# A fused attention and two-expert-layer kernel: ranks behind the second product, row numbers last, and attention's small steps at other places

## The chip, the cores and the metric

The program runs on one core of a Trainium2 chip. The metric is device time in microseconds (us) of one execution. Engines: PE is the matrix engine (TensorE), DVE is VectorE, ACT is ScalarE, POOL is GpSimd, SP is SyncE, which here only issues DMAs.

## The reference

Three stages run one after the other on 3072 tokens (4 batches of 768) of width 384 (8 heads of 48).

```
f = sigmoid(f_logit)                                  # gated linear attention, per head
state = f[t,:,None] * state + k[t] (x) v[t];  y[t] = q[t] @ state
x = y as rows of 384                                  # first expert layer
logits = normalised x @ normalised expert_emb.T / tau; e = argmax; gate = softmax(logits)[e]
x = gate * (relu(x @ w1[e]) @ w2[e])                  # 8 experts, w1 384x1024, w2 1024x384
skip rows with x @ w_skip <= 0                        # second expert layer: router w_gate,
out = x + gate * (relu(x @ w1b[e]) @ w2b[e])          # else as the first; skipped rows stay x
```

## The kernel before

**Engines and waits.** Each engine runs its own instruction list, written out by hand; semaphores (wait_ge, then_inc) are the only order between engines. An engine that waits holds up all that stands behind it in its list.

**Attention** works on 16 pairs of heads (g = 4b + hp; b is the batch, hp the pair in it), each in a head part and a tail part. PE transposes k, q and f, makes scores (L732) and sums (L718), and multiplies by state (L745) and scores (L753). DVE does the decays (L1171 to L1173, L1184, L1186), k_up (L1179), q_down (L1189) and the running state (L1211). ACT copies and exponentiates. POOL masks the scores (L557), lays out carry (L564), which the state of the next pair needs, and makes the low parts of weights (L550). Between the pairs lies the routing of the batch before. In the tail of hp = 1 DVE normalises and picks the expert (L1273 to L1278: maximum, shifted, tie, first index, onehot_b), and stands there ahead of q_down. In the head of hp = 2 PE counts the ranks (L797 to L802). Then DVE makes row numbers (slot_idx, L1303), and POOL sends the rows to sorted_rows in HBM, by one indirect DMA for each of six chunks (L571). A safety count (ps_safe, L707 and L1208) tells all engines whether a slower exact path must run; with these data it doesn't.

**Weights.** All products of the expert layers are made from a high part (w_hi, ACT, L969) and a low part (w_lo = raw_w - w_hi, POOL, L550) of both operands. The weights of one expert (3 MB) are eight slices of 128x768. There are two buffers. SP loads expert 0 early in attention. Its eight slices are made there, one a pair, in pairs 2, 3, 4, 5, 8, 9, 12 and 13 (first_slice). SP then loads expert 2 into the same buffer, and expert 1 into the other when attention is done, as that buffer lies on attention's memory.

**An expert layer** (m = 0, then m = 1) goes over the experts and over tiles of 128 sorted rows (27 tiles in the first layer, mostly 3 to an expert). One tile on PE, in its order: transposes of xs (L924), the first half of the second product of the tile before (contract, L871 to L873), its router logits (L895), transposes of its second hidden half (L880), the first half of the first product (expand, L861 to L863), **rank of the tile before** (L797, L802), the second half of its second product (contract), transposes of the first hidden half, two thirds of the second half of expand, transposes of row_out of the tile before (route_t, L889), the rest. On DVE: x_lo (L1474), then old_tile of the tile before, which is route_a (L1427 to L1434, its end is onehot_b), hidden_low (h_lo, L1480), place_a (L1442 to L1455: send_row, out_idx, then slot_idx and next_slot from the ranks), finish_a (L1418, L1419: row_out), and last h_lo of the first half of this tile, which the next tile's contract on PE needs. On POOL: two w_lo slices of the next expert, the sends of the tile before (L602, L605), two more slices, and the confirmation that the sends landed, which frees send_row. Slices 0 to 3 fall in an expert's first tile, 4 to 7 in its second, so that four stand in a row from the one tile to the next.

## Time and profile before

| | |
|---|---|
| runs before, us | 795.44, 790.67, 786.24 (median 790.67) |
| profiled execution | 786.7 us, of which 785.0 us are the span of its instructions |
| PE / DVE / ACT / POOL busy, share of span | 89% / 50% / 45% / 50% |
| mean granted clock of TensorE | 0.936 of full |
| attention | 0 to 206 us |
| last routing, plan, first rows back | 206 to 231 us |
| first expert layer | 231 to 537 us |
| its end, plan, first rows back | 537 to 561 us |
| second expert layer | 561 to 785 us |

The span begins with the program's first instruction, and 1.7 us of the time lie outside of it. Busy PE is not the same as PE at its peak: the same instructions take longer where the granted clock is at 0.50 (1.2 GHz) than at 1.00 (2.4 GHz).

### The profile page before, as it was taken

What the parts mean: (1) busy time and instruction counts of PE and PEld (TensorE: products, weight loads), DVE (VectorE), ACT (ScalarE), POOL (GpSimd) and SP (SyncE); (2) the same over time, 40 slices, a digit from 0 to 9 for tenths busy, and PEclk for the clock granted to TensorE, in tenths of its full rate; (3) what the DMA queues carried; (4) which work ended last, traced back from release to release, by engine and by line L of the source; (5) the groups of instructions that cost most, each with busy time, mean ns of one, the idle gap of its engine ahead of it and who ended that gap; (6) DMA issues with size and microseconds to landing.
All of it is one profiled execution on the core that took longest, in us unless ns stands there. A gap on an engine that the chain in (4) does not pass through costs nothing.

```text
span 785.0 us, 16547 instructions
## 1 busy us (share of the span) xinstructions
PE 698.8 (89%) x4912; PEld 628.4 (80%) x4913; DVE 388.7 (50%) x1001; ACT 355.7 (45%) x611; POOL 388.7 (50%) x309
## 2 busy tenths in 40 slices
PE   5889998998719999999999999998399999999992
PEld 4889897997718888788888888887289899898992
DVE  5858988987223554564455555554222222222220
ACT  3556565573205535353534544532254544545420
POOL 4234473543147456563553746641377556658610
PEclk9999999998559999999999999999599999999997
DMA  8675476556530334261423333510454744744110
GB/s 154 158 200 113 83 171 121 129 116 208 188 107 18 126 111 154 86 201 40 134 89 107 129 128 109 179 52 21 152 180 152 228 140 146 229 151 145 51 41 21
DMA packets 147048, 99.42 MB, mean 127 GB/s; under 512 B 109983, under 2 KB 137930, under 8 KB 147008
## 3 DMA queue, kind: packets, MB, share of 16 engines
q1 hardware_dynamic: 140544, 86.19, 38.8%
q0 software_dynamic: 6464, 12.72, 4.5%
q8 instruction: 22, 0.36, 0.2%
q14 instruction: 18, 0.15, 0.1%
HBM read 83.00 MB, written 23.14 MB: 135 GB/s over the span
## 4 chain that ended last, share of the span: by engine, by line
PE 74%; DVE 9%; issue 8%; DMA 3%; ACT 2%; POOL 1%; SPq 1%; ACTq 0%; POOLq 0%; DVEq 0%
PE banks_y L871 9%; PE banks_y L873 8%; PE bank_a L861 8%; PE banks_y L872 8%; PE bank_a L862 8%; PE bank_a L863 8%; PE bank_b L880 5%; PE banks_y L753 4%; PE banks_s L924 2%; PE banks_s L732 2%; PE banks_y L895 2%; PE banks_y L745 2%; DMA raw_f<-in_f_logit 1%; PE banks_y L682 1%; PE banks_s L654 1%
## 5 line engine op out<-in xcount | busy, mean ns | idle before, releaser
L550 POOL TENSOR_TENSOR w_lo<-raw_w,w_hi 128x768 fp32r<-128x768 f32 x128 | 234.0, 1856 | 75.0 <-ACT w_hi L969 68.0
L871 PE MATMUL banks_y<-w_hi,h_hi 128*128 128x384 f32 x384 | 136.4, 355 | 4.7 <-DVE h_lo L1480 4.7
L873 PE MATMUL banks_y<-w_hi,h_lo 128*128 128x384 f32 x384 | 130.5, 340 | 0.0
L872 PE MATMUL banks_y<-w_lo,h_hi 128*128 128x384 f32 x384 | 130.1, 339 | 0.0
L861 PE MATMUL bank_a<-w_hi,x_hi 128*128 128x512 f32 x288 | 127.2, 442 | 3.0 <-DVE x_lo L1474 3.0
L862 PE MATMUL bank_a<-w_lo,x_hi 128*128 128x512 f32 x288 | 115.9, 402 | 0.0
L863 PE MATMUL bank_a<-w_hi,x_lo 128*128 128x512 f32 x288 | 115.8, 402 | 0.0
L1094 ACT ACTIVATE h_hi<-bank_b 128x512 fp32r<-128x512 f32 x96 | 57.4, 598 | 127.7 <-PE bank_b L880 126.5
L1090 ACT ACTIVATE hid<-bank_a 128x512 f32<-128x512 f32 x96 | 57.5, 599 | 106.0 <-PE bank_a L863 104.7
L969 ACT ACTIVATE w_hi<-raw_w 128x768 fp32r<-128x768 f32 x128 | 101.0, 838 | 3.0 <-DMA raw_w<-in_moe_w 3.0
L1480 DVE TENSOR_TENSOR h_lo<-bank_b,h_hi 128x512 fp32r<-128x512 f32 x96 | 66.2, 689 | 61.2 <-ACT h_hi L1094 60.4
L1474 DVE TENSOR_TENSOR x_lo<-banks_s,x_hi 128x384 fp32r<-128x384 f32 x48 | 26.7, 557 | 124.1 <-ACT x_hi L1127 124.1
L602 POOL DMA_INDIRECT sorted_rows<-send_row,slot_idx x28 | 27.7, 989 | 113.1 <-DVE slot_idx L1454 113.1
L871 PEld LDWEIGHTS banks_y<-w_hi,h_hi 128*128 128x128 f32 x384 | 72.7, 189 | 8.0 <-DVE h_lo L1480 6.3
L872 PEld LDWEIGHTS banks_y<-w_lo,h_hi 128*128 128x128 f32 x384 | 72.9, 190 | 0.7
L873 PEld LDWEIGHTS banks_y<-w_hi,h_lo 128*128 128x128 f32 x384 | 72.7, 189 | 0.0
L557 POOL TENSOR_SCALAR_AFFINE_SELECT scores<-scores 128x768 f32<-128x768 f32 x32 | 33.1, 1035 | 78.0 <-ACT scores L1002 78.0
L863 PEld LDWEIGHTS bank_a<-w_hi,x_lo 128*128 128x128 f32 x288 | 55.4, 192 | 13.7
L861 PEld LDWEIGHTS bank_a<-w_hi,x_hi 128*128 128x128 f32 x288 | 55.9, 194 | 12.3 <-DVE x_lo L1474 4.5
L862 PEld LDWEIGHTS bank_a<-w_lo,x_hi 128*128 128x128 f32 x288 | 56.1, 195 | 7.7
L880 PE MATMUL bank_b<-ident,hid 128*128 128x128 f32 x384 | 59.9, 279 | 1.4 <-ACT hid L1090 1.4
L880 PEld LDWEIGHTS bank_b<-ident,hid 128*128 128x128 f32 x384 | 48.8, 149 | 5.2 <-ACT hid L1090 2.8
(183 smaller groups left out, 1105.7 us busy)
## 6 DMA issues: line engine op xcount, KB each, us to landing
raw_w<-in_moe_w SPq DMA_DIRECT2D x32, 1536.0 KB, 7.0
xs<-sorted_rows SPq DMA_DIRECT2D x48, 194.0 KB, 5.1
raw_f<-in_f_logit SPq DMA_DIRECT2D x32, 144.0 KB, 2.7
raw_k<-in_k SPq DMA_DIRECT2D x32, 144.0 KB, 2.9
raw_q<-in_q SPq DMA_DIRECT2D x32, 144.0 KB, 3.1
raw_v<-in_v SPq DMA_DIRECT2D x32, 144.0 KB, 2.9
kept<-sorted_rows SPq DMA_DIRECT2D x21, 194.0 KB
sorted_rows<-pad_row SPq DMA_DIRECT2D x16, 194.0 KB, 2.4
```

The lines of the kernel that those rows point to most:

```text
L550: pool.tensor_tensor(w_lo[par][:, sl, :], raw_w[par][:, sl, :], w_hi[par][:, sl, :].bitcast(F32), ALU.subtract).then_inc(w_split_lo, 1)
L861: pe.matmul(ps_h[half], x_hi[:, kd, :], hi, start=(kd == 0), stop=False)
L862: pe.matmul(ps_h[half], x_hi[:, kd, :], lo, start=False, stop=False)
L863: ins = pe.matmul(ps_h[half], x_lo[:, kd, :], hi, start=False, stop=(kd == KD - 1))
L871: pe.matmul(ps_out, h_hi[:, kf, :], hi, start=(kf == 0), stop=False)
L872: pe.matmul(ps_out, h_hi[:, kf, :], lo, start=False, stop=False)
L873: ins = pe.matmul(ps_out, h_lo[:, kf, :], hi, start=False, stop=(kf == KF - 1))
L880: ins = pe.transpose(ps_ht[half][:, j * P:(j + 1) * P], hid[:, half * HALF + j * P:half * HALF + (j + 1) * P], ident[:])
L969: act.activation(w_hi[par][:, sl, :], raw_w[par][:, sl, :], ACT.Copy).then_inc(w_split_hi, 1)
L1090: act.activation(hid[:, half * HALF:(half + 1) * HALF], ps_h[half], ACT.Relu).then_inc(s[f"relu{half}"], 1)
L1094: act.activation(h_hi[:, half * (KF // 2):(half + 1) * (KF // 2), :].rearrange("p k x -> p (k x)"), ps_ht[half], ACT.Copy).then_inc(s[f"h_ ...
L1480: dve.tensor_tensor(h_lo[:, hs, :].rearrange("p k x -> p (k x)"), ps_ht[half], h_hi[:, hs, :].bitcast(F32).rearrange("p k x -> p (k x)"), ...
```

## The change

Nothing is added or taken away in what is computed; steps are put at other places.

- **First expert layer.** PE makes the second half of the second product ahead of the ranks, not behind them. On DVE the onehot goes behind h_lo, out of route_a into place_a; the row numbers become a function of their own, place_slot, that stands behind finish_a; next_slot is made ahead of slot_idx. PE's router logits now also wait for place_slot of the tile before, as both use one bank. The semaphore of row numbers starts at one, so POOL waits for u + 2 in place of u + 1 (the same event).
- **Attention.** The high slices go to pairs 3, 4, 7, 8, 11, 12, 14, 15, the low ones to 3, 4, 8, 12, and the last four to the end, ahead of the last batch's sends. SP loads expert 1 ahead of expert 2. The six sends of a batch stand as 2 behind carry (hp = 2), 2 between the masks and 2 behind carry (hp = 3), in place of 3 and 3 ahead of carry. The norm of the expert embedding (ACT and DVE, pair 1) is begun earlier. The safety count moves behind the sums of the last pair and into another bank.

```diff
@@ order in the program, pools and waits @@
-        ps_safe = bank_y[0:1, 448:449]
+        ps_safe = bank_a[0:1, 448:449]
...
-            return g - 2 if b == 0 and hp >= 2 else 2 * b + hp if b > 0 and hp < 2 else None
+        HI_PAIRS = (3, 4, 7, 8, 11, 12, 14, 15)
+        LO_PAIRS = (3, 4, 8, 12)
@@ SP @@
+            sp.wait_ge(y_ready, PAIRS)
+            load_w1(0, 1, 1)
+            load_w2(0, 1, 1)
             wait_split(sp, 0, 2)
             load_w1(0, 2, 0)
             load_w2(0, 2, 0)
-            sp.wait_ge(y_ready, PAIRS)
-            load_w1(0, 1, 1)
-            load_w2(0, 1, 1)
@@ POOL @@
                 mask(g, 0)
+                if b > 0 and hp == 3:
+                    send_chunks(b - 1, (2, 3), (b - 1) % 2)
                 mask(g, 1)
-                if b > 0 and hp >= 2:
-                    send_chunks(b - 1, range((hp - 2) * (C // 2), (hp - 1) * (C // 2)), (b - 1) % 2)
-                if first_slice(g) is not None:
-                    split_lo(0, 0, first_slice(g))
+                if g in LO_PAIRS:
+                    split_lo(0, 0, LO_PAIRS.index(g))
                 if g + 1 < PAIRS:
                     carry_decay(g + 1)
+                if b > 0 and hp >= 2:
+                    send_chunks(b - 1, (0, 1) if hp == 2 else (4, 5), (b - 1) % 2)
+            for sl in range(len(LO_PAIRS), SLICES):
+                split_lo(0, 0, sl)
             send_batch(B - 1, (B - 1) % 2)
@@ PE @@
-                if last:
-                    pe.wait_ge(safe_ready, 1)
-                    pe.matmul(ps_safe, safe_b[:], ones[:, 0:1], start=True, stop=True).then_inc(safe_summed, 1)
...
                 else:
+                    pe.wait_ge(safe_ready, 1)
+                    pe.matmul(ps_safe, safe_b[:], ones[:, 0:1], start=True, stop=True).then_inc(safe_summed, 1)
                     logits(KD * B - 2, ps_logit_end)
...
                     pe.wait_ge(g["xt_copied"], k + 1)
+                    pe.wait_ge(g["slot"], k + 1)
...
+                    pe.wait_ge(s["h_lo1"], u + 1)
+                    contract(par, 1).then_inc(s["y"], 1)
                     if m == 0:
                         rank(g, u + 1, 1, ps_rank_1, ps_count_1)
-                    pe.wait_ge(s["h_lo1"], u + 1)
-                    contract(par, 1).then_inc(s["y"], 1)
@@ ACT: emb_sq in the head of pair 1, its root ahead of the wait for y_ready; split_hi in HI_PAIRS @@
...
@@ DVE @@
             def place_a(ch, k):
+                first_i, valid = cols[:, 1, 0:1], cols[:, 4, 0:1]
                 dve.tensor_scalar(onehot_b[:, 0, :], order[:, 0, :], first_i, valid, ALU.is_equal, ALU.mult).then_inc(g["onehot"], 1)
...
+            def place_slot(ch, k):
+
+                g = gs[1]
                 dve.wait_ge(g["onehot"], k + 1)
                 dve.wait_ge(g["rank"], k + 1)
...
+                ch.link(dve.tensor_tensor(next_slot[:, 0, :], next_slot[:, 0, :], ps_count_1[:, 0, :], ALU.add))
                 dve.tensor_scalar(slot_idx[:, 0:1], cols[:, 3, 0:1], BIG, None, ALU.add).then_inc(g["slot"], 1)
-                ch.link(dve.tensor_tensor(next_slot[:, 0, :], next_slot[:, 0, :], ps_count_1[:, 0, :], ALU.add))
...
                         hidden_low(1, u)
                         place_a(ch, u)
                         finish_a(ch, u)
+                        place_slot(ch, u)
```

How the instructions stand in a row, at the three places that matter. DVE, first expert layer, a tile's work for the tile before, in the kernel before (cols holds the small columns, tie the marks of the best expert):

```order
L1433 TENSOR_REDUCE cols<-tie 128x1
...
L1434 TENSOR_SCALAR onehot_b<-order,cols 128x8
L1480 TENSOR_TENSOR h_lo<-bank_b,h_hi 128x512
L1442 TENSOR_SCALAR cols<-cols 128x1
...
L1446 COPY send_row<-row_out 128x388
...
L1451 TENSOR_TENSOR slot_e<-banks_y,next_slot 128x8
...
L1454 TENSOR_SCALAR slot_idx<-cols 128x1
...
L1419 TENSOR_SCALAR row_out<-banks_y,kept 128x384
```

The same piece of the changed kernel:

```order
L1488 TENSOR_TENSOR h_lo<-bank_b,h_hi 128x512
L1444 TENSOR_SCALAR onehot_b<-order,cols 128x8
L1446 TENSOR_SCALAR cols<-cols 128x1
...
L1450 COPY send_row<-row_out 128x388
...
L1423 TENSOR_SCALAR row_out<-banks_y,kept 128x384
L1459 TENSOR_TENSOR slot_e<-banks_y,next_slot 128x8
...
L1462 TENSOR_TENSOR next_slot<-next_slot,banks_y 128x8
...
L1463 TENSOR_SCALAR slot_idx<-cols 128x1
```

The onehot has moved behind h_lo, and the row number behind row_out. On POOL, the pairs 5, 6 and 7 of attention with carry of the next pair behind each, before:

```order
L557 AFFINE_SELECT scores<-scores 128x768 x2
L550 TENSOR_TENSOR w_lo<-raw_w,w_hi 128x768
L564 COPY carry<-decay 128x48x5
L557 AFFINE_SELECT scores<-scores 128x768 x2
L571 DMA sorted_rows<-rows,slot_idx 25600x388 x3
L564 COPY carry<-decay 128x48x5
L557 AFFINE_SELECT scores<-scores 128x768 x2
L571 DMA sorted_rows<-rows,slot_idx 25600x388 x3
L564 COPY carry<-decay 128x48x5
```

and after:

```order
L555 AFFINE_SELECT scores<-scores 128x768 x2
L562 COPY carry<-decay 128x48x5
L555 AFFINE_SELECT scores<-scores 128x768 x2
L562 COPY carry<-decay 128x48x5
L569 DMA sorted_rows<-rows,slot_idx 25600x388 x2
L555 AFFINE_SELECT scores<-scores 128x768
L569 DMA sorted_rows<-rows,slot_idx 25600x388 x2
L555 AFFINE_SELECT scores<-scores 128x768
L562 COPY carry<-decay 128x48x5
L569 DMA sorted_rows<-rows,slot_idx 25600x388 x2
```

The slice of pair 5 is gone, and carry stands ahead of the sends. On POOL at the end of attention, after (before, nine sends stood there in a row behind the last masks, three of batch 2 and six of batch 3, and no slice):

```order
L569 DMA sorted_rows<-rows,slot_idx 25600x388 x2
L548 TENSOR_TENSOR w_lo<-raw_w,w_hi 128x768 x4
L569 DMA sorted_rows<-rows,slot_idx 25600x388 x6
```

Four slices now stand between the masks of the last pair and the sends of the last batch.

## Rows read from the trace of the kernel before

**Rows 1.** Windows: stretch, length, busy by engine, granted clock, DMA share, GB/s.

```profile
0.00:206.00 206.00, 184.59 (x2030) 173.86 (x2031) 156.69 (x257) 109.92 (x161) 88.99 (x106) 0.93 0.61 141
206.00:231.00 25.00, 5.18 (x33) 4.50 (x33) 7.92 (x41) 2.69 (x6) 5.84 (x6) 0.50 0.54 193
231.00:537.00 306.00, 291.48 (x1683) 256.66 (x1682) 157.67 (x547) 140.62 (x275) 166.18 (x116) 0.98 0.33 108
138.65:142.06 3.41, 3.41 (x19) 3.41 (x19) 3.24 (x7) 0.81 (x1) 1.51 (x3) 0.50 0.05 19
```

**Rows 2.** Waits: who waited for whom, us in total, times, longest.

```profile
PE banks_y L797 <- DVE onehot_b L1434: 10.7, 8, 1.4
PE banks_s L732 <- DVE q_down L1189: 5.9, 4, 1.8
```

**Rows 3.** Windows of single tiles, from one tile's xs transposes to the next's.

```profile
262.71:273.45 10.74, 10.74 (x65) 9.60 (x64) 5.87 (x21) 6.56 (x12) 5.80 (x5) 1.00 0.58 200
273.45:287.78 14.33, 12.60 (x65) 11.15 (x64) 7.65 (x21) 6.44 (x12) 11.12 (x8) 0.88 0.43 141
343.99:356.73 12.74, 11.01 (x66) 9.63 (x65) 7.65 (x21) 6.44 (x12) 9.53 (x7) 1.00 0.48 154
```

**Rows 4.** Timeline of POOL and DVE, tiles that begin at 262.71 and 273.45.

```profile
265.50 3.64 POOL L550 TENSOR_TENSOR w_lo<-raw_w,w_hi 128x768 fp32r<-128x768 f32 x2 [3.71 <-ACT w_hi L969]
266.93 0.43 DVE L1434 TENSOR_SCALAR onehot_b<-order,cols 128x8 bf16<-128x8 f32 x1
268.25 1.11 DVE L1446 COPY send_row<-row_out 128x388 f32<-128x388 f32 x1
273.25 7.21 POOL L550 TENSOR_TENSOR w_lo<-raw_w,w_hi 128x768 fp32r<-128x768 f32 x4
277.54 2.95 DVE L1434 TENSOR_SCALAR onehot_b<-order,cols 128x8 bf16<-128x8 f32 x1
```

**Rows 5.** Timeline, the same tiles: send, row_out, h_lo, PE behind them, h_hi.

```profile
270.97 0.99 POOL L602 DMA_INDIRECT sorted_rows<-send_row,slot_idx  x1 [1.83 <-DVE slot_idx L1454]
271.04 0.62 DVE L1419 TENSOR_SCALAR row_out<-banks_y,kept 128x384 f32<-128x384 f32 x1
271.85 0.69 DVE L1480 TENSOR_TENSOR h_lo<-bank_b,h_hi 128x512 fp32r<-128x512 f32 x1 [0.19 <-issue]
272.43 0.49 PE L889 MATMUL banks_s<-ident,row_out 128*128 128x128 f32 x3
273.70 0.42 PE L871 MATMUL banks_y<-w_hi,h_hi 128*128 128x384 f32 x1
277.12 0.60 ACT L1094 ACTIVATE h_hi<-bank_b 128x512 fp32r<-128x512 f32 x1 [1.03 <-PE bank_b L880]
```

**Rows 6.** Groups of the first layer: instructions, then busy us, mean ns, idle before.

```profile
L1452 DVE TENSOR_TENSOR slot_e<-slot_e,onehot_b 128x8 f32<-128x8 f32 x26 | 4.3, 167 | 0.9
```

**Rows 7.** Timeline of attention: tie beside POOL's slice (pair 5), and tie alone.

```profile
80.92 1.85 POOL L550 TENSOR_TENSOR w_lo<-raw_w,w_hi 128x768 fp32r<-128x768 f32 x1 [0.36 <-ACT w_hi L969]
81.13 1.70 DVE L1276 SCALAR_TENSOR_TENSOR tie<-shifted,order 128x48 f32<-128x48 f32 x1
214.43 0.21 DVE L1276 SCALAR_TENSOR_TENSOR tie<-shifted,order 128x48 f32<-128x48 f32 x1
```

**Rows 8.** Timeline of attention: pair 7's state, the last pair's safety count.

```profile
101.39 0.76 DVE L1211 TENSOR_TENSOR_SCAN state<-banks_y,carry 128x288 f32<-128x288 f32 x1 [1.42 <-POOL carry L564]
190.46 0.17 PE L707 MATMUL banks_y<-ones,safe_b 128*1 128x1 bf16 x1 [0.75 <-DVE safe_b L1336]
```

**Rows 9.** Timeline of pair 2: the embedding's transposes and the next f.

```profile
36.02 0.32 PE L810 MATMUL banks_y<-ident,emb_n 8*128 8x8 f32 x3 [2.18 <-DVE emb_n L1244]
46.56 1.51 PE L654 MATMUL banks_s<-ident,raw_f 128*128 128x128 f32 x6 [2.91 <-DMA raw_f<-in_f_logit]
```

**Rows 10.** Timeline of the first layer's end.

```profile
546.99 0.97 POOL L605 DMA_INDIRECT out<-send_row,out_idx  x1 [0.30 <-issue]
550.82 0.36 DVE L1446 COPY send_row<-row_out 128x388 f32<-128x388 f32 x1
```

More of the change, by code:

```diff
@@ L249, in gla_moe_program @@
         from_one_act = [y_copied, exact_copied]
-        from_one_dve = [exact_done, gs[0]["slot"], gs[0]["onehot"], exact_gs["slot"], exact_gs["onehot"]] + [
+        from_one_dve = [exact_done, gs[0]["slot"], gs[0]["onehot"], exact_gs["slot"], exact_gs["onehot"], gs[1]["slot"]] + [
             f[n] for f in fs for n in ("x_lo", "row")]
@@ L598, in send_routed @@
             def send_routed(u):
-                pool.wait_ge(gs[1]["slot"], u + 1)
+                pool.wait_ge(gs[1]["slot"], u + 2)
                 settle(pool)
@@ L820, in _ @@
             pe.wait_ge(gs[0]["logit_read"], KD * B - 1)
+            pe.wait_ge(safe_known, 1)
             logits(KD * B - 1, ps_logit_end)
@@ L990, in pair_head @@
                     guess_decay(g + 1)
+                if g == 1:
+                    act.wait_ge(small_in, 32 + 32 * KD)
+                    act.activation(emb_sq[:], emb_rows[:], ACT.Square, accum_out=en[:, 0:1]).then_inc(emb_sq_ready, 1)
             def copy_x(r):
@@ L1019, in pair_tail @@
                     square(g - 1)
-                if first_slice(g) is not None:
+                if g in HI_PAIRS:
                     act.wait_ge(w1_in[0], 16)
                     act.wait_ge(w2_in[0], 16)
-                    split_hi(0, 0, first_slice(g))
+                    split_hi(0, 0, HI_PAIRS.index(g))
                 if f_next:
@@ L1027, in pair_tail @@
                     copy_x(x_part(g))
+                if g == 1:
+                    act.wait_ge(emb_norm_ready, 1)
+                    ach.link(act.activation(en[:, 2:3], en[:, 1:2], ACT.Ln))
+                    act.activation(en[:, 3:4], en[:, 2:3], ACT.Exp, scale=0.5).then_inc(emb_sq_ready, 1)
                 act.wait_ge(y_ready, g + 1)
@@ L1033, in pair_tail @@
                                ACT.Copy).then_inc(y_copied, 1)
-                if g == 1:
-                    act.wait_ge(small_in, 32 + 32 * KD)
-                    act.activation(emb_sq[:], emb_rows[:], ACT.Square, accum_out=en[:, 0:1]).then_inc(emb_sq_ready, 1)
-                    act.wait_ge(emb_norm_ready, 1)
-                    ach.link(act.activation(en[:, 2:3], en[:, 1:2], ACT.Ln))
-                    act.activation(en[:, 3:4], en[:, 2:3], ACT.Exp, scale=0.5).then_inc(emb_sq_ready, 1)
             def root(s, b):
@@ L1161, in _ @@
             ROUTE_A = 19
-            TILE_STEPS = (10, 1)
+            TILE_STEPS = (11, 1)
             starts = lambda t: t[:].rearrange("p (c x) -> p c x", c=C)[:, :, 0]
@@ L1205, in pair_head @@
                     place_ranks(ch, gs[0], b - 1)
-                if last:
-                    dve.wait_ge(safe_summed, 1)
-                    dve.tensor_copy(safe_count[:], ps_safe).then_inc(safe_known, 1)
                 dve.wait_ge(u_ready, g + 1)
@@ L1217, in pair_tail @@
                     scale_k(ch, g + 1, 1 - par)
+                if g == 1:
+                    dve.wait_ge(emb_sq_ready, 1)
+                    dve.tensor_scalar(en[:, 1:2], en[:, 0:1], TINY, None, ALU.max).then_inc(emb_norm_ready, 1)
                 if hp == 1 and b > 0:
@@ L1228, in pair_tail @@
                     add_logits(ch, KD * B - 2, ps_logit_end)
+                    dve.wait_ge(safe_summed, 1)
+                    dve.tensor_copy(safe_count[:], ps_safe).then_inc(safe_known, 1)
                 if g == 1:
@@ L1433, in route_a @@
                 ch.link(dve.tensor_reduce(first_i, tie[:, 0, :], AX.X, ALU.min))
-                dve.tensor_scalar(onehot_b[:, 0, :], order[:, 0, :], first_i, valid, ALU.is_equal, ALU.mult).then_inc(g["onehot"], 1)
             def place_a(ch, k):
                 g, total = gs[1], cols[:, 2, 0:1]
-                valid = cols[:, 4, 0:1]
+                first_i, valid = cols[:, 1, 0:1], cols[:, 4, 0:1]
+                dve.tensor_scalar(onehot_b[:, 0, :], order[:, 0, :], first_i, valid, ALU.is_equal, ALU.mult).then_inc(g["onehot"], 1)
                 dve.wait_ge(g["exp"], k + 1)
@@ L1446, in place_a @@
                 dve.tensor_copy(send_row[:], row_out[:])
-                dve.scalar_tensor_tensor(out=out_idx[:], in0=valid, scalar=BIG, in1=row_out[:, TOKEN:TOKEN + 1],
-                                         op0=ALU.mult, op1=ALU.add)
+                ch.link(dve.scalar_tensor_tensor(out=out_idx[:], in0=valid, scalar=BIG, in1=row_out[:, TOKEN:TOKEN + 1],
+                                                 op0=ALU.mult, op1=ALU.add))
+            def place_slot(ch, k):
+                g = gs[1]
                 dve.wait_ge(g["onehot"], k + 1)
@@ L1511, in _ @@
                     place_a(ch, last)
+                    place_slot(ch, last)
                     make_plan(ch, 1)
```

4 lines of the change are left out of this document (removed).

## Prediction

> **What bounds the kernel now.** I read the stages first, then who waits for whom, then single tiles. In attention PE is busy 185 of 206 us, in the first expert layer 291 of 306 us [rows 1], so PE is the bound in both, and what the change can win there is PE's idle time and its time at the low clock. Between the two lie 25 us in which PE does little. In the second expert layer the order is as before, and I count nothing. Two waits carry the rest: PE's ranks for the onehot, 10.7 us in 8 times, and the scores for q_down, 5.9 us in 4 times [rows 2]. A usual tile of the first layer takes 10.74 us, a second tile of an expert 12.74 us, and 14.33 us where the clock falls after the wait [rows 3].
>
> **Why the onehot is late.** It takes 0.43 us in a first tile and 2.95 us in a second [rows 4]; the second case comes seven times. The reader is to see where it ends: at 277.54 + 2.95 = 280.49, while POOL's four w_lo slices run from 273.25 to 280.46. The slices are four of 1.8 us, so it began 0.7 us into the third, was not let in at that one's end (278.66), and was held until the fourth's. In the first tile it began 0.4 us before the first of two slices ended and got in there (267.36); the copy into send_row was then held until the second ended (269.14, and it ended at 269.36). So DVE's onehot and send_row wait for POOL's slices, whereas h_lo doesn't. In the order before, h_lo stands behind the onehot, and PE waits for both.
>
> **Second tiles, seven times.** With the new order h_lo needs only h_hi, which ends at 277.72 [rows 5], so it is done by 278.4, ahead of PE, which comes to the ranks at 279.1 or so. The 2.0 us of wait (12.74 - 10.74) go. What is late next? place_slot is five linked steps of 0.2 us [rows 6], and now stands behind row_out. So the row number comes some 2.3 us later than before, and POOL's sends, which follow it, begin at about 273.5 in place of 270.97 [rows 5] and end at about 275.8. The four slices shift with them, to 275.8 to 283.0, with ends at 277.6, 279.4, 281.2 and 283.0. The onehot begins at 278.4, 0.8 us into the second slice, nearest to the case at 277.54. By that row it is held through the third (281.2). send_row then begins at 281.6 and is held to 283.0, and row_out, which in a usual tile ends 8.95 us after the tile's start (271.66 for 262.71), ends at 284.2, 10.8 us after it. PE wants row_out for route_t 9.7 us after the start (272.43) and waits 1.1 us. Behind row_out come place_slot and h_lo, which PE wants 11.0 us after the start (273.70); that is late by another 0.3 us. The new stall is 1.4 us, the gain 0.6 us a tile, **4.2 us** in seven. The ends of this: 0.1 us a tile if the onehot is held to the last slice's end, 2.0 us if DVE is let in at every end, so 0.7 to 14 us. Two of the seven stalls are followed by a stretch at the low clock, 14.33 - 12.74 = 1.6 us each; I take one of them as gone, **1.6 us** (0 to 3.2).
>
> The Trainium skill (SBUF — State Buffer, "Who interferes with whom") says that VectorE in a 2-port mode and GpSimd lock each other out for the whole instruction, and that the one that issues first has the ports. By that rule the onehot would get in at 278.66. The row of 2.95 us speaks against it, and the row of 0.43 us for it; by the rule alone the gain would be the full 14 us. It is the first rival below.
>
> **Other tiles, 19 of them.** h_lo of the first half begins 0.81 us after row_out began (271.04, 271.85) and is done at 272.54; PE wants it at 273.70. place_slot pushes it by 0.85 us, to 273.4 [rows 5, 6]. That leaves 0.3 us, and costs nothing. If place_slot took more, each tile would pay.
>
> **The layer's end.** place_slot of the last tile but one now comes after row_out, so its two sends go out 2.8 us later than at 546.99 (the first of them starts 1.3 us ahead) [rows 10]. Their landing frees send_row, which DVE writes at 550.82. The send at 546.99 could take until then, 3.8 us, and 2.3 us are near what lies between; with 549.8 + 2.3 the copy starts at 552.1 or later. Plan and first rows follow, and the new order of next_slot adds 0.2: **-1.6 us** (0 to -2.8).
>
> **Attention, pairs 5, 9 and 13.** tie takes 1.70 us beside POOL's slice and 0.21 us alone [rows 7], and stands ahead of q_down, for which PE then waits 1.8 us, three times [rows 2]. No slice stands there in the changed kernel: 3 x 1.49 = **4.5 us**. All of DVE's steps shift with it, state too, so nothing takes the wait's place. Each of these waits is followed by 3.41 us at half the clock (one is the last of [rows 1]), which cost up to 1.7 us each. In two of the three pairs DVE's state ends as late as PE's slowed work, so only one is paid in full: I take **2.0 us** (0 to 5.1). The slices that move to pairs 3, 7, 11, 14 and 15 lie on ACT, which is busy 110 of 206 us [rows 1]; without that cover one would cost its 0.83 us.
>
> **Smaller ones.** Carry ahead of the sends: DVE sat idle 1.42 us for it in pair 7 [rows 8], of which PE saw little; 0.4 us (0 to 1.4). The sends between the masks hold the second mask by under 1 us, and PE comes to it later still. The safety count: PE waited 0.75 us for it [rows 8], and won't: 0.75 us. The embedding's norm: PE's 2.18 us in pair 2 go [rows 9], but 10 us later PE waits 2.91 us for f, which sits in SP's queue behind 3 MB of weights and lands at 46.4 whatever PE did. So PE only waits 5 us there in place of 2.9, and this edit is worth **0** (0 to 2.2). Expert 2's weights are now loaded after attention, behind those of expert 1. Each pair of transfers takes about 10 us, so they end near 225, when the first rows are written; between 206 and 231 the DMA engines are busy 0.54 [rows 1]. I take -0.3 us (0 to -8, the latter if the padding row, which is on SP's queue behind them, has to wait for all of them). The four slices at the end run from 203 to 210, before DVE's last tie at 214.43 [rows 7].
>
> **The sum.** 4.2 + 1.6 - 1.6 + 4.5 + 2.0 + 0.4 + 0.75 - 0.3 = 11.55 us. The profiled execution took 786.7, so 775.2; it lies 4.0 us under the median of 790.67, which would make it 779.1. The clock's low stretches fall otherwise in each execution, and the three runs before spread over 9 us. I take the middle, **777**, with its own range from 771 to 783.
>
> **Rivals.**
> - POOL lets DVE in at each slice's end. For it: 0.43 us for the onehot of a first tile [rows 4]. Then no second tile waits, 7 x 1.4 = 9.8 us more: 767. Chance 0.2.
> - DVE is let in only when POOL has no slice left. For it: the 2.95 us ended where the run of four did. Then ranks wait until 283.0 and all but 0.1 us a tile of the stall stays: 777 + 3.5 = 780.5. Chance 0.15.
> - The wins in attention are lost at its end: expert 2's 3 MB hold up the padding row and the first rows. For it: f behind the weights in pair 2, 2.91 us of wait [rows 9]. Against: half of the DMA engines' time is free there [rows 1]. 777 + 7 = 784. Chance 0.12.
> - Slower: h_lo of the first half comes late in every tile of the first layer. Place: PE's contract at 273.70. It decides from the point at which place_slot takes over 1.2 us in place of 1.0, as where its product of slot_e and onehot, with two operands in SBUF as tie has, is held by a slice. At 1.8 us, one slice, 26 tiles lose up to 0.8 us each, 21 us: 798. Against: in most tiles POOL has no slice at that time, as it waits for the same row number. Chance 0.06.
> - The change does nothing that shows, PE being busy 95% of the layer: 787. Chance 0.07.
>
> My forecast has 0.4. The range takes in the first and the third rival and leaves 0.1 on either side: 765 to 787. A measurement of this kernel tells about 1% from no change, 7.9 us, so faster means under 782.8. Of the forecast's 0.4 nearly all is faster, with the first rival, most of the second and a little of the third: 0.73; slower 0.06, the rest the same.
>
> **What would show it.** Right: tie at 0.21 us in pairs 5, 9, 13, and no wait of 1.8 us for q_down; PE's wait for the onehot gone, and one of about 1.1 us for row_out in its place in the second tiles, at a period near 12.1 us; send_row longer there. A longer wait for f in pair 2. Usual tiles still at 10.74 us. Wrong: usual tiles over 10.8 us (h_lo late), second tiles at 10.7 or 12.7 us, first rows later than 25 us after attention.

## The result, and the profile after

The changed kernel takes **810.6 us** (median of four runs, 806.8 to 813.6) against 792.9 us for the kernel before on the same chip: a ratio of 1.023 (95% interval 1.015 to 1.032). By the interval it is slower, by 1.5 to 3.2%; whether by 2% or more four runs don't settle. I had forecast 777 us. The profiled execution took 810.9 us. (Ratios are of undisturbed runs and so may differ a little from the quotient of two medians.)

The stages of the changed kernel, in windows as in [rows 1] (attention; to the first tile; first layer without its last 23.5 us):

```profile
0.00:215.00 215.00, 194.97 (x2030) 184.67 (x2031) 149.15 (x257) 109.50 (x161) 81.89 (x104) 0.87 0.54 121
215.00:242.00 27.00, 4.94 (x31) 4.23 (x31) 9.53 (x41) 2.80 (x6) 10.28 (x9) 0.50 0.80 293
242.00:561.50 319.50, 294.69 (x1691) 257.96 (x1692) 179.85 (x548) 140.96 (x276) 165.88 (x114) 0.98 0.32 103
```

Each stage is longer: attention by 9 us at a clock of 0.87 in place of 0.93, the routing by 2, the layer by 13.5 at the same clock. PE's waits (in total, times, longest), against [rows 2]:

```profile
PE banks_s L927 <- DMA xs<-sorted_rows: 29.0, 2, 17.4
PE banks_s L656 <- DMA raw_f<-in_f_logit: 11.9, 2, 6.8
PE banks_s L891 <- DVE row_out L1423: 10.8, 7, 2.6
PE banks_y L798 <- DVE onehot_b L1444: 8.9, 4, 4.5
PE banks_y L873 <- DVE h_lo L1488: 8.2, 7, 1.5
PE banks_y L746 <- DVE state L1212: 3.7, 4, 1.1
PE banks_s L733 <- DVE q_down L1193: 1.7, 4, 0.8
```

The wait for q_down has gone as forecast, but that for the onehot is nearly as large as before, and others have grown: row_out from 1.0 us to 10.8, h_lo from 4.7 to 8.2, state from 1.7 to 3.7. A usual tile and two of the long ones, against [rows 3]:

```profile
262.34:273.00 10.66, 10.66 (x65) 9.61 (x64) 5.52 (x21) 3.56 (x8) 5.63 (x5) 1.00 0.09 20
283.85:298.48 14.63, 11.13 (x66) 9.54 (x65) 11.08 (x26) 6.44 (x12) 11.76 (x8) 1.00 0.41 135
321.85:339.70 17.85, 13.39 (x65) 11.54 (x64) 12.20 (x22) 6.44 (x12) 13.57 (x10) 0.81 0.36 117
```

**Where the layer's time goes.** In the second of these DVE is busy 11.1 us with 26 instructions, in the first 5.5 us with 21. The timeline there, from the sends ahead of it (start, length, in brackets the idle time before):

```profile
274.14 0.98 POOL L607 DMA_INDIRECT out<-send_row,out_idx  x1 [0.30 <-issue]
274.86 0.01 SPq L386 DMA_DIRECT2D raw_w<-in_moe_w  x1
...
282.64 3.61 POOL L548 TENSOR_TENSOR w_lo<-raw_w,w_hi 128x768 fp32r<-128x768 f32 x2 [7.52 <-issue]
282.82 1.68 DVE L1460 TENSOR_TENSOR slot_e<-slot_e,onehot_b 128x8 f32<-128x8 f32 x1
...
285.82 0.41 PE L873 MATMUL banks_y<-w_hi,h_hi 128*128 128x384 f32 x1 [1.48 <-DVE h_lo L1488]
...
290.55 1.82 DVE L1444 TENSOR_SCALAR onehot_b<-order,cols 128x8 bf16<-128x8 f32 x1
292.66 1.98 DVE L1450 COPY send_row<-row_out 128x388 f32<-128x388 f32 x1
294.56 1.77 DVE L1451 SCALAR_TENSOR_TENSOR out_idx<-cols,row_out 128x1 uint32<-128x1 f32 x1
...
297.39 0.55 PE L891 MATMUL banks_s<-ident,row_out 128*128 128x128 f32 x3 [2.02 <-DVE row_out L1423]
```

Read it downwards. The send to out begins 1.14 us *after* the tile's start at 273.00; before, the send at 260.82 began 1.9 us ahead of the tile at 262.71. SP's load of 1.5 MB of weights follows 0.7 us later. POOL then stands idle until the sends have landed, 7.5 us, so the first slices of an expert come 9.6 us into its first tile, not 2.8 [rows 4]. There they meet four small DVE instructions: slot_e's product, the onehot, send_row's copy and out_idx (0.17, 0.28, 0.36 and 0.15 us elsewhere). Each is held, that is, it ends only with a slice, and PE waits twice. How long the send took to land, in the lists of DMA issues (last column, us), in the changed kernel:

```profile
out<-send_row,out_idx POOLq DMA_INDIRECT x1, 7.0
```

and in the kernel before, the send at 260.82:

```profile
out<-send_row,out_idx POOLq DMA_INDIRECT x1, 2.4
```

In another expert (the tile of 17.85 us) the onehot starts 0.07 us ahead of four slices in a row and is held by all four:

```profile
327.00 7.25 DVE L1444 TENSOR_SCALAR onehot_b<-order,cols 128x8 bf16<-128x8 f32 x1
327.07 7.14 POOL L548 TENSOR_TENSOR w_lo<-raw_w,w_hi 128x768 fp32r<-128x768 f32 x4
...
334.32 0.19 PE L798 MATMUL banks_y<-onehot_b,before 128*128 128x8 bf16 x1 [4.46 <-DVE onehot_b L1444]
```

In seven second tiles it took 1.82, 7.25, 1.83, 4.97, 1.80, 3.69 and 1.84 us: it got in after one, four, one, three, one, two and one slices. In the four cases of one, POOL itself stood idle behind that slice, for 0.03 to 0.44 us; the runs that let it in after two, three and four slices had no such gap.

**Where attention's time goes.** PE now waits 6.85 us for f in pair 2, and from inside that wait on the clock is at 1.2 GHz for 20.5 us (PE is busy 15.5 of them). Timeline, and a window of that stretch:

```profile
47.65 1.51 PE L656 MATMUL banks_s<-ident,raw_f 128*128 128x128 f32 x6 [6.85 <-DMA raw_f<-in_f_logit]
```

```profile
42.65:63.13 20.48, 15.48 (x98) 14.84 (x100) 5.87 (x8) 5.36 (x7) 1.44 (x2) 0.50 0.59 134
```

The ties are short, against [rows 7], and in the next pair PE waits for state instead:

```profile
179.98 0.21 DVE L1280 SCALAR_TENSOR_TENSOR tie<-shifted,order 128x48 f32<-128x48 f32 x1
...
187.99 1.34 PE L746 MATMUL banks_y<-state,q_down 64*128 64x48 f32 x20 [1.06 <-DVE state L1212]
```

The last four slices run across the end of attention (215.24), and only then may SP load expert 2:

```profile
212.26 7.11 POOL L548 TENSOR_TENSOR w_lo<-raw_w,w_hi 128x768 fp32r<-128x768 f32 x4
219.39 0.37 SPq L386 DMA_DIRECT2D raw_w<-in_moe_w  x1
...
239.78 0.37 SPq L474 DMA_DIRECT2D xs<-sorted_rows  x1
```

### The profile page after: what moved, and what is told of

The parts are those of the page before. It is cut to its first block, busy times and chain, and to the rows that moved or that the text cites. A ratio compares the mean times of both kernels' runs of the same rounds, so it can differ in the third digit from the quotient of the medians.

```text
span 808.9 us, 16634 instructions
## 1 busy us (share of the span) xinstructions
PE 709.6 (88%) x4912; PEld 638.3 (79%) x4913; DVE 404.1 (50%) x1001; ACT 355.2 (44%) x611; POOL 386.8 (48%) x309
## 4 chain that ended last, share of the span: by engine, by line
PE 69%; DVE 13%; issue 7%; DMA 5%; ACT 2%; SPq 1%; POOL 1%; ACTq 0%; POOLq 0%; DVEq 0%
PE banks_y L873 7%; PE banks_y L875 7%; PE banks_y L874 7%; PE bank_a L863 7%; PE bank_a L864 7%; PE bank_a L865 7%; PE banks_y L754 5%; PE bank_b L882 5%; DMA out<-send_row,out_idx 3%; DVE onehot_b L1444 3%; PE banks_s L733 2%; PE banks_y L746 2%; PE banks_y L684 2%; PE banks_s L927 2%; PE banks_y L898 2%
## 5 line engine op out<-in xcount | busy, mean ns | idle before, releaser
L873 PE MATMUL banks_y<-w_hi,h_hi 128*128 128x384 f32 x384 | 134.0, 349 | 8.3 <-DVE h_lo L1488 8.2
L873 PEld LDWEIGHTS banks_y<-w_hi,h_hi 128*128 128x128 f32 x384 | 72.7, 189 | 14.2 <-issue 7.9
L864 PEld LDWEIGHTS bank_a<-w_lo,x_hi 128*128 128x128 f32 x288 | 56.2, 195 | 7.7
L754 PE MATMUL banks_y<-raw_v,scores 128*128 128x48 f32 x384 | 55.9, 303 | 0.0
```

The lines of the kernel that those rows point to most:

```text
L754: ins = pe.matmul(ps_y[h][:, c, :], scores[:, half, h * (C // 2) + c3, :], raw_v[par][:, c, h, :], start=False, stop=True, skip_group_chec ...
L864: pe.matmul(ps_h[half], x_hi[:, kd, :], lo, start=False, stop=False)
L873: pe.matmul(ps_out, h_hi[:, kf, :], hi, start=(kf == 0), stop=False)
```

## The experiments

One table serves all. "Attention" is the start of ACT's copy of the last pair's rows; "low" is the time until then at 1.2 GHz; "rows" is from there to the first tile's xs transposes, and "layer" from those to the second layer's first ones. All four are from the one profiled execution, in us; the ratio, to the kernel before on the same chip, is of all runs.

| kernel | attention | low | rows | layer | ratio (95% interval) |
|---|---|---|---|---|---|
| before | 206.2 | 30.0 | 24.5 | 329.9 | 1 |
| changed | 215.2 | 56.5 | 27.0 | 342.8 | 1.023 (1.015 to 1.032) |
| e1 layer only | 217.8 | 57.2 | 24.7 | 340.6 | 1.019 (1.012 to 1.026) |
| e2 attention only | 215.1 | 56.7 | 27.0 | 327.7 | 1.006 (1.002 to 1.011) |
| e3 changed, weights behind sends | 211.5 | 45.2 | 27.0 | 513.3 | 1.248 (1.240 to 1.255) |
| e4 before, order in PSUM | 206.9 | 32.9 | 24.6 | 315.3 | 0.979 (0.970 to 0.987) |
| e5 e2, expert 2 first | 217.4 | 57.8 | 30.3 | 330.2 | 1.008 (1.003 to 1.012) |
| e6 e2, norm as before | 217.9 | 60.1 | 26.9 | 327.8 | 0.998 (0.992 to 1.004) |
| e7 e1, number ahead of row_out | 206.0 | 29.6 | 24.5 | 333.9 | 1.002 (0.998 to 1.006) |
| e8 e1, weights behind last sends | 208.7 | 37.8 | 24.7 | 338.4 | 1.016 (1.006 to 1.026) |
| e9 changed, order in PSUM | 214.9 | 56.2 | 27.1 | 328.2 | 1.011 (1.006 to 1.015) |
| e10 before, f ahead of weights | 213.3 | 52.2 | 24.6 | 327.8 | 0.996 (0.993 to 1.000) |
| e11 three edits | 200.6 | 26.4 | 24.8 | 312.1 | 0.959 (0.955 to 0.964) |
| e12 e11, sends and safety moved | 204.2 | 39.9 | 24.4 | 315.5 | 0.970 (0.965 to 0.975) |
| e13 before, number last alone | 212.9 | 42.9 | 24.5 | 354.5 | 1.043 (1.035 to 1.051) |
| e14 e11, safety moved | 200.0 | 28.0 | 24.6 | 311.3 | 0.961 (0.955 to 0.967) |
| e15 e11, sends moved | 202.8 | 36.8 | 24.6 | 311.6 | 0.968 (0.963 to 0.974) |
| e16 e11, slices at hp = 0 | 206.0 | 43.5 | 24.6 | 311.7 | 0.970 (0.964 to 0.976) |

The layer's span holds time at the low clock too, so two layers that differ by 2 or 3 us need not differ in their waits. What PE stands idle there, from the first tile's start to the last one's, tells more: 14.5 us before, 24.6 in the changed kernel, 22.6 in e1, 2.2 in e4, 14.2 in e7, 17.6 in e8, 14.7 in e9 and 29.2 in e13.

**The two halves of the change (e1, e2).** The diff of each is that half of the change's diff.

> The kernel before with the change of the first expert layer alone; attention, SP's weights and the safety count stay. Theory (two separate losses, the layer's being 13 us, the span from the first xs transposes of the first layer to those of the second, 342.8 us against 329.9): the layer takes 340 to 345 us here, attention 206 us, the time is 10 to 14 us above the kernel before. Rival 1 (the layer is slow only because attention leaves it with late weights or a late start): the layer takes 330 to 333 us and the time is within 3 us of before. Rival 2 (my prediction, second tiles 0.6 us shorter): 4 us below before.

> The kernel before with the change of attention alone (weight slices, SP's order, sends, embedding norm, safety count); the first expert layer stays. Theory (PE's waits in pair 2, gathered into one of 6.85 us ahead of f, are followed by 20 us at the low clock and eat the gain of the ties): attention ends at 210 to 216 us in place of 206, the rows of the first tile come 2.4 us later still, the layer takes 330 us; the time is 5 to 12 us above before. Rival 1 (the low clock in pairs 2 to 6 of the one profile was chance): attention ends at 198 to 203 us and the time is 3 to 8 us below before. Rival 2 (my prediction): 7.35 us below.

The layer alone costs 10.7 us in the layer, and by the ratio some 15 us in all, a little more than expected; attention alone loses 5 us, the lower end of what I expected. The table also shows why attention must not be read off one profile: e1's attention is that of the kernel before, and ended 11.7 us later, with 27.2 us more at the low clock. That is 0.43 us for each us at the low clock. (The profiled execution of e1 is the longest of its four; the other five profiles of this attention, by themselves, give 0.49.) Taken off at 0.43, the six profiles of the old attention (before, e1, e4, e7, e8, e13) end at 192.4 to 194.5 us, and the five of the changed one at 190.7 to 192.5 (changed, e2, e9, e3, e5). So its instructions and waits are shorter by an estimate of 1.8 us (0.6 to 3 for rates from 0.35 to 0.5); what it loses is clock.

**Is it the landing? (e3, e8)**

```diff
@@ e3: SP, load_next, in all tiles of the first layer @@
+                        if m == 0:
+                            sp.wait_ge(rows_free[0], t + 1)
@@ e8: the same place, on the kernel of e1, ahead of each load of weights @@
+                                sp.wait_ge(rows_free[0], t)
```

> The changed kernel, with one wait more: in the first layer SP issues the loads of weights only once the sends of the tile before have landed (the count that frees send_row). Theory (the sends come 2.3 us later than before and now share the queues with 1.5 MB of weights, so they land after 7.0 us in place of 2.3, POOL's slices wait for them, and fall on the product for the row number, 1.68 us in place of 0.17, and on the onehot, 1.8 to 7.3 us): sends land after 2 to 3 us in every tile, first slices of an expert begin 4 to 5 us after its first tile in place of 9.6, the wait of 1.48 us for h_lo at the start of second tiles goes, and the time is 4 to 10 us below the changed kernel. Rival (the order on DVE itself costs it, not the landing): the sends land early but the second tiles still take 14 us and the time is that of the changed kernel within 3 us.

> The kernel before with the change of the first layer, and SP issues an expert's weights only once the sends that begin at the start of the same tile have landed (one tile earlier than in the run whose weights waited for the sends of the tile itself, where xs was held up 11 us). Theory (landing of 7 us in place of 2.3 starts the chain: late slices, then stretched row numbers and onehots): the sends land after 2.0 to 3.0 us everywhere, the first slices of an expert begin 3.5 to 5 us after its first tile in place of 9.6, the stretched product of 1.68 us at the start of second tiles goes, and the layer takes 328 to 334 us in place of 340.6. Rival (the order on DVE itself costs it): 338 us or more although the sends land early. A cost of its own: xs is issued behind the weights, at 5 us, and may be late by 0 to 1 us in first tiles.

In e3 the wait was for sends that start 11 us into the same tile, so xs, which stands behind the weights in SP's queue, came 11 us late in two tiles of each expert. The sends did land within 2.1 to 2.6 us in nearly all tiles, but the time says nothing of the theory. e8 waits for the sends at the tile's start. They landed after 2.1 to 2.8 us in most tiles and 3.7 at most, and the first slices of an expert began 4.8 to 6.1 us into its first tile. The layer gained only 2.2 us on e1: the theory expected 7 to 12. With the landing short, the four slices stand in one run again, in the second tile, and the onehot (start, length) is held by them for longer than in the kernel before:

```profile
313.23 7.22 POOL L555 TENSOR_TENSOR w_lo<-raw_w,w_hi 128x768 fp32r<-128x768 f32 x4
...
315.56 4.92 DVE L1446 TENSOR_SCALAR onehot_b<-order,cols 128x8 bf16<-128x8 f32 x1
```

PE waited 15.0 us for the onehot in e8. But its waits for row_out and h_lo all but went, and PE's idle time fell by 5.0 us of the 8.1 that e1 adds, though xs was late once, by 1.3 us. The layer hardly shows it, as it ran 8 us longer at the low clock (34.6 in place of 26.6), an estimate of 3.4 us at 0.43. So the long landing is more than half of the idle time that the layer's change adds. The rest comes with a late send even where it lands fast: POOL's run of four slices ends 7.0 us into a second tile in the kernel before, and 10.1 us in e8, and the onehot with it. Both parts go back to the late send.

**Which move makes the send late? (e7, e13)**

```diff
@@ e7: DVE, on the kernel of e1 @@
+                        place_slot(ch, u)
                         finish_a(ch, u)
-                        place_slot(ch, u)
@@ e13: DVE, on the kernel before (ranks and onehot stay; place_slot with its waits as in the change) @@
                         place_a(ch, u)
                         finish_a(ch, u)
+                        place_slot(ch, u)
```

> The kernel before with the change of the first layer, but with the row number ahead of row_out on DVE (not last). The sends then start 0.8 us earlier than in the change, 1.4 us later than before: 0.3 us after a tile's start in place of 1.14. Theory (the sends' landing runs into the weights' load, issued 1.2 us after the start of an expert's first tile): still late, landing after 4 to 7 us, second tiles 13 to 15 us, the layer 336 to 342 us. Rival (the row number in last place is what costs, by h_lo and the send behind it): the layer takes 326 to 332 us.

> The kernel before with one edit in the first layer: the row number behind row_out on DVE; ranks and onehot stay where they were. With all of the layer's change the layer takes 340.6 us, with the number ahead of row_out 333.9, before 329.9. Theory (the number in last place delays the sends and puts its product, the first-half h_lo and the slices in each other's way): 333 to 338 us, sends start 0.5 to 1 us later than before, the landing of one expert's sends runs into the weights in some tiles. Rival (the number in last place costs only with the ranks behind the second product, since only then does the send come after a tile's start): 329 to 332 us.

The row number in last place alone costs 24.6 us in the layer, far more than I expected; without it the other two moves cost 4.0, with no more idle time of PE than before, and the ratio of 1.002 can't tell it from nothing. finish_a waits for the whole second product, so behind it the number can't come before the tile's end. In e13 PE's waits, and a send, 11.3 us after the start of its tile at 249.19 (8.5 in the same tile before, and 7.5 in a usual one):

```profile
PE banks_y L797 <- DVE onehot_b L1435: 11.9, 12, 2.6
PE banks_y L871 <- DVE h_lo L1485: 11.6, 20, 1.5
...
PE banks_s L889 <- DVE row_out L1420: 7.2, 6, 3.7
```

```profile
260.51 0.99 POOL L602 DMA_INDIRECT sorted_rows<-send_row,slot_idx  x1 [5.71 <-DVE slot_idx L1460]
```

In e7 the send to out began 0.9 us earlier than in e1 (0.2 in place of 1.1 us after a tile's start) and took 2.1 to 2.6 us to land in nearly every tile; the landings of 7 us are gone, and the run of slices ends 8.4 us into a second tile. The theory had it still late: wrong. The layer's 333.9 lie between what the two expected. Moving ranks and onehot gives back 14 us where the number is last (354.5 to 340.6), and gains nothing where it isn't.

**Is it the ports? (e4, e9)** h_lo, x_lo and row_out read one operand from PSUM and were never seen stretched. So the onehot gets order from there:

```diff
+        ps_order = bank_y[:, 400:400 + E]
@@ make_plan(0) @@
+                    ch.link(dve.tensor_copy(ps_order, order[:, 0, :]))
@@ route_a @@
-                dve.tensor_scalar(onehot_b[:, 0, :], order[:, 0, :], first_i, valid, ...
+                dve.tensor_scalar(onehot_b[:, 0, :], ps_order, first_i, valid, ...
```

(e9 on the changed kernel, in bank_u and behind the wait for the exponent, as ACT reads that bank.)

> The kernel before, with one operand of the first layer's onehot (order, 128x8) read from a PSUM bank in place of SBUF, as h_lo, x_lo and row_out have one operand there and are never seen stretched beside POOL's slices. Theory (a DVE instruction is held by POOL's slices only if all it touches is in SBUF): the onehot takes 0.15 to 0.35 us in second tiles in place of 2.95, PE's wait for it goes, second tiles take 10.7 to 11 us in place of 12.73, the time is 12 to 18 us below before. Rival 1 (held whatever its operands, since its output or its columns are in SBUF): 2.95 us stay, same time. Rival 2 (the stall moves to send_row and row_out, which is held by the rest of the four slices): onehot short, PE waits 1 to 2 us for row_out instead, 0 to 5 us below before.

> The changed kernel, with one operand of the first layer's onehot read from PSUM, as in the kernel before with order in PSUM. Theory (of the layer's 13 us the onehot, held through POOL's run of slices, is half; the rest is held too: the product for the row number, 1.7 us, and send_row and out_idx, 1.7 to 2.0 us each, all with operands in SBUF alone): PE's waits for the onehot (4.46, 2.17, 0.90 us) go, those of 1.5 us for h_lo and some 2 us for row_out stay, the layer takes 332 to 338 us in place of 342.8, the time is 5 to 10 us below the changed kernel's 810.56. Rival 1 (all of it hangs on the onehot, as in the order before): 314 to 320 us. Rival 2 (what is not held at the onehot is held at send_row instead): 340 to 343 us.

e4 did what the theory said, 17.0 us by the ratio. The onehot beside the same four slices:

```profile
275.07 7.24 POOL L551 TENSOR_TENSOR w_lo<-raw_w,w_hi 128x768 fp32r<-128x768 f32 x4
...
279.37 0.29 DVE L1437 TENSOR_SCALAR onehot_b<-banks_y,cols 128x8 bf16<-128x8 f32 x1
```

0.29 us in place of 2.95 [rows 4], and all second tiles take 10.7 to 11.0 us. The Trainium skill (SBUF — State Buffer, "Who interferes with whom") says that a VectorE instruction with at most one SBUF input, outside the 2-port modes, does not contend with GpSimd; this row agrees. e9 gained 14.6 us in the layer, as e4 did (14.6), a little more than expected (7.8 us less at the low clock are in it, some 3 us), and there the change's 12.9 us stay whole, with 12.5 us more of idle time than in e4: PE waits for instructions behind other held ones.

```profile
PE banks_y L874 <- DVE h_lo L1491: 10.0, 10, 1.5
PE banks_s L892 <- DVE row_out L1426: 6.5, 3, 3.8
```

**Attention's parts (e5, e6, e10).** e5 loads expert 2 ahead of expert 1 again; e6 puts the norm back; e10 is the kernel before with expert 0's weights behind f, k and q of pair 4:

```diff
@@ e5: SP, on e2 @@
             wait_split(sp, 0, 2)
             load_w1(0, 2, 0)
...
             sp.wait_ge(y_ready, PAIRS)
             load_w1(0, 1, 1)
@@ e10: SP @@
-            load_w1(0, 0, 0)
-            load_w2(0, 0, 0)
...
+            load_pair(4, 0, v_used=3, between=first_weights)
@@ e10: pairs of the eight slices @@
+        SLICE_PAIRS = (3, 3, 4, 5, 8, 9, 12, 13)
```

> The kernel before with the change of attention, but with SP's weights as before (expert 2 as soon as the buffer is free, expert 1 behind attention). Theory (the 3 MB of expert 2 behind attention hold up the padding row and the first rows): the first xs transposes come 24.3 to 24.8 us after the last pair's rows, in place of 27.0, and the time is 2 to 3 us below that of the attention change alone (792.6). Rival (the 2.4 us come from the four slices ahead of the last sends): 27 us stay.

> The kernel before with the change of attention, but with the norm of the expert embedding where it was. Theory (one wait of 6.8 us ahead of f lets the clock fall for 13 to 20 us; in two shorter ones it falls for less): PE waits 2.2 and 3 us, the low stretch is 3.4 to 10 us, pairs 2 and 3 take 29 to 31 us together in place of 35.6, and the time is 2 to 6 us below that of the attention change alone (792.6). Rival (the stretch is chance: the layer's change alone showed 17.07 us behind its waits of 2.17 and 2.49 us, at the norm's old place): pairs 2 and 3 take 31 to 35 us, same time within 2 us.

> The kernel before, with SP's load of expert 0 behind f, k and q of pair 4 in place of ahead of them, and the slices in pairs 3, 3, 4, 5, 8, 9, 12 and 13. Theory (PE's wait for f in pair 2 is the 3 MB ahead of it in SP's queue, and the clock falls behind it for 3.4 to 20 us): no wait for f, no low stretch near 45 us, attention ends 3 to 7 us earlier than 206 to 209 us, time 3 to 7 us below before. Rival (the weights only push another load: k, q or v of pair 4 or 5, or pair 3's slices wait for them): a new wait of 2 us or more by 60 us, same time.

e5: 30.3 us, worse. The load of expert 2 waits for the last slices wherever it stands, and here expert 1 waits behind it. The slices at the end are the cause; with all of them inside attention again (e11, e12) the first rows come after 24.4 to 24.8 us, in e12 with the change's sends. That they act through the load fits the times of issue: in the changed kernel the padding row goes out 16.7 us after attention's end (16.2 before), but xs 7.8 us behind it (5.9 before). e6: PE waits 2.17 and 4.81 us, and 17.1 us at the low clock follow all the same; pairs 2 and 3 take 35.5 us against e2's 35.6. The rival holds in the profile. The ratio came out lower than e2's, by 0.8% with intervals that overlap, so a small cost of the early norm stays open. e10: the wait for f is gone, and the stretch near 45 us, but attention ended at 213.3, with 17 us at the low clock in pairs 6 and 7. The theory was right on the wait and wrong on the end; by the ratio the time is 3 us lower (0 to 6).

**A version that beats both (e11), and around it (e12, e14, e15, e16).**

```diff
@@ e11: the edits of e4 and e10, with @@
+        SLICE_PAIRS = (3, 3, 4, 4, 7, 8, 11, 12)
@@ e16 @@
+        SLICE_PAIRS = (3, 3, 4, 4, 8, 8, 12, 12)
```

e14 adds the change's place of the safety count to e11, e15 that of the sends, e12 both.

> The kernel before with three edits: the onehot's operand in PSUM (alone 17 us), f ahead of expert 0's weights, and the slices of pairs 5, 9 and 13 moved to 4, 7 and 11, so that no tie stands beside one. Sends, safety count, norm and the order of the first layer are as before. Theory (the moved slices were the part of the change that was right: three ties of 1.70 us become 0.21, three waits for q_down of 1.8 us become 0.3): attention ends at 196 to 202 us, the time is 760 to 768 us. Rival (freed time of DVE goes into the wait of 1.07 us for state in pairs 6, 10 and 14, as in the changed kernel, and the clock falls elsewhere): attention ends at 203 us or later, the time is that of the onehot alone, 770 to 773 us.

> The same three edits, and with them the change's places of the sends behind carry and between the masks, and of the safety count; norm and SP's order as before. Theory (these two are worth 0 to 1 us; the change's first rows came late by its last four slices and expert 2's load behind attention, not by the sends): within 3 us of the run with the three edits, first xs transposes 24 to 25 us after attention. Rival 1 (the safety count's new place or the sends bring the low stretch of 58 us in pairs 14 and 15 that all runs of the change's attention showed, against 44 to 48 us): 2 to 4 us above it. Rival 2 (carry ahead of the sends pays): 1 to 3 us below it.

> The run with the three edits (757.4 us) with the safety count at the place of the change. With the sends' places as well it took 766.8 us. Theory A (the safety count: PE's stop of 0.7 to 0.9 us for it in pair 15's head goes, but the clock then falls one pair earlier): 763 to 768 us, low stretch of 54 us or more from pair 14 on. Theory B (the sends): 755 to 759 us, pairs 14 and 15 take 28 to 29.5 us.

> The run with the three edits (757.4 us) with the sends at the places of the change (two behind carry, two between the masks, two behind carry). Theory A (it is the safety count that costs): 756 to 759 us. Theory B (the sends: the ones between the masks hold the second mask and with it PE's products of scores, the ones behind carry hold the next mask): 763 to 768 us, with a low stretch from pair 14 on. Rival C (neither: the clock's fall there is chance and differs between programs): both runs lie between 758 and 765.

> The run with the three edits, with the slices of pairs 7 and 11 in pairs 8 and 12 (two in one pair, none at hp = 3). There state waited 0.41 us in pairs 7 and 11, behind POOL's slice and sends. Theory (that wait goes): 1 us less, 755.5 to 757 us. Rival (two slices in a row on POOL or ACT in pairs 8 and 12 hold a mask or the scores there): a new wait of 0.5 to 1.5 us twice, 758 to 760 us.

e11 takes 757.4 us, 4.1% below before. Its f is issued at 38.18 and the weights at 42.28, and PE doesn't wait for it:

```profile
38.18 1.13 SPq L366 DMA_DIRECT2D raw_f<-in_f_logit  x2
42.28 0.55 SPq L388 DMA_DIRECT2D raw_w<-in_moe_w  x1
```

e14 measured 759.5 and e15 764.8 us: by the numbers set, the sends cost and the safety count hardly does. But e16 touches neither and measured 766.7. What e12, e15 and e16 share is the clock in pairs 14 and 15, in windows of e11 and of e16:

```profile
171.42:200.57 29.15, 26.03 (x249) 24.16 (x247) 14.84 (x32) 10.14 (x16) 11.65 (x12) 0.78 0.48 160
```

```profile
172.05:205.98 33.93, 32.35 (x249) 30.46 (x247) 14.85 (x32) 10.23 (x15) 11.68 (x12) 0.61 0.41 138
```

The same 249 instructions, 4.8 us apart, with PE busy longer and a clock of 0.61 against 0.78. Less the low clock at 0.43, e12, e15 and e16 end attention at 187.0 to 187.3 us and e11 at 189.2 (it has waits of 0.41 us for state in pairs 7 and 12 that they lack). By this estimate they have fewer waits, and are slower. What starts the long stretch is not settled: all five have the same waits of 0.3 and 1.07 us in pair 14.

## Why the prediction was wrong, step by step

- **Second tiles, predicted +4.2 us (and +1.6 for the clock): wrong, and it is the step that decides.** The send's time was right: 273.5 - 262.71 = 10.8 us after the tile's start forecast, 10.5 measured (272.85 - 262.34). What I took for granted was its landing. I wrote that "the four slices shift with them, to 275.8", 2.4 us into the second tile. But landing took 7.0 us in place of 2.3: an expert's first slices came at 9.6 us of its first tile in place of 2.8, and the next at 4.8 us of the second (288.69 - 283.85). I had the weights' load at 264.0 in the profile before, ahead of which the sends just got through, and didn't ask what a later send meets. That is more than half of it. Where the landing is short (e8: slices at 2.9 us into the second tile, 2.4 forecast) the step still fails at its second half: the onehot was not "held through the third", but for all of the rest of the run, and PE waited 2.1 us, not 1.4.
- **"Other tiles ... costs nothing": right for usual tiles (10.67 us), wrong where slices are late.** h_lo of the first half was late by 1.5 us at the start of three experts' second tiles, and by 0.4 at a fourth's, since the product ahead of it took up to 1.68 us. That was the mechanism of the slower rival (798 us, chance 0.06), which I put aside as POOL "waits for the same row number" then. It did not: the late slices were waiting for the landing.
- **The layer's end, -1.6 us: right.** The last stretch takes 33.96 us against 32.45.
- **The ties, +4.5 us: right in mechanism, wrong in size.** They take 0.21 us and the wait for q_down fell from 1.8 to 0.3. But I wrote that "nothing takes the wait's place", and a wait of 1.07 us for state stands in pairs 6, 10 and 14 in all profiles with free ties: 3 x (1.5 - 1.07) = 1.3 us, less where the old order had that wait too. All waits together made attention some 1.8 us shorter (0.6 to 3), where my terms had 5.65.
- **Low clock behind those waits, +2.0 us: wrong in sign.** The three short stretches went, and longer ones came: 56 us in place of 30, 11 us at 0.43. Since the old attention showed 30 to 57 us too, I can't say how much of it is the change's; e2's ratio puts all of attention and the first rows at 5 us slower (1 to 8).
- **The norm, 0, by a wait of 5 us: the wait was 6.85.** PE came 2.85 us earlier, as forecast, but f landed 1.1 us later, not at the same time "whatever PE did". Its price stays open (e6).
- **Expert 2's weights, -0.3 (to -8): mis-sized, 2.4 us.** The load does stand ahead of the first rows, as the third rival had it, but put there by the last slices, not by SP's order (e5).
- **Carry and safety count, +1.15:** worth nothing that the time shows (e14, e12); with the change's sends e15 is 7 us slower than e11, but e16, without them, is slower by as much.

Of the rivals, "DVE is let in only when POOL has no slice left" was nearest for the runs of four, but the rows show one to four slices. The layer's 10.7 to 12.9 us and e2's 5 make 16 to 18, against the 17.7 between the medians.

## What to carry to other kernels

When a step moves later, follow its DMA to its landing: ask what is issued in the 2 us behind the new place, and who stands still until it has landed. A small instruction on VectorE with all its operands in SBUF can take as long as a whole run of GpSimd's (7.25 us here); one operand in PSUM was worth more here than any order (17 us). Compare stages at an equal clock before explaining a difference between single profiles.

## What the runs showed of the hardware

- A send by indirect DMA landed in 2.1 to 2.7 us when it began 1.4 us or more ahead of a 1.5 MB load from another queue, in 6.5 to 7.5 us when it began 0 to 0.8 us ahead of it (once, at 0.74 us, in 2.2), in 5.8 to 5.9 us when it began 1.5 us behind it (four times), and in 3.7 to 4.6 us when it began 3 to 4 us behind it.
- A VectorE instruction held by POOL's back-to-back instructions got in after one, two, three or four of them (1.8 to 7.25 us). Where POOL paused between two of them it got in there; what picks a place in a run without a pause is not settled. Held were the onehot, send_row's copy, and forms with two operands in SBUF (slot_e, out_idx, tie); with an operand in PSUM none was (h_lo stayed at 0.69 us, x_lo at 0.56, row_out at 0.62, and the onehot of e4 at 0.29).
- One program's attention spent between 30 and 57 us at 1.2 GHz in six profiles, and ended between 206 and 218 us accordingly; 1 us at the low clock cost 0.43 to 0.49 us.
